# Routing search of an expert network: nine steps for ten, 24 small counting matmuls in the first round, and a new order of VectorE's work in the expert loop

## The chip, the cores and the metric

The kernel runs on one core of one Trainium2 chip. The metric is the device time of one execution in microseconds (us). TensorE (PE) multiplies matrices, with its weight loads shown apart as PEld; VectorE (DVE), ScalarE (ACT) and GpSimd (POOL) do the elementwise work; SyncE (SP) issues most DMAs. Each engine works through its own queue in order, and the queues are tied by semaphores that the program sets and waits for.

## What is computed

Three layers follow one another. A gated linear attention (4 batches, 8 heads, 768 tokens, head size 40) gives x with 3072 rows of 320. A router gives every token one of 8 experts with room for 384 tokens each:

```python
logits = x @ w_gate
order = np.argsort(-logits.flatten())
for idx in order:
    tok, e = (int(idx) // E, int(idx) % E)
    if assigned[tok] >= 0 or counts[e] >= cap:
        continue
    assigned[tok] = e
    counts[e] += 1
for e in range(E):
    mask = assigned == e
    out[mask] = np.maximum(x[mask] @ w1[e], 0.0) @ w2[e]
```

The last layer is the same for all tokens: h = x @ w_in (320 to 2048), g = max(h, 0) + alpha * min(h, 0), y = g @ w_out. All of it is in float32; the large products are made from three matmuls on a high and a low part of each operand.

## The kernel before

**Attention, then a first routing round, then eight experts.** The tokens lie in NT = 24 tiles of 128, T = 4c + b. Attention goes over these tiles. After it the router's greedy order is turned into rounds. A round finds the next expert that becomes full, with its 384 tokens. Round 0 runs alone, before the first expert; round e + 1 runs beside expert e, spread over its hidden tiles. In a round every token has a best open expert; its logit is held as two integers in floats, `route_value` (high bits) and `route_tie` (low bits and the token's place), and `best` finds the maximum of each over the 8 experts and writes the one-hot `choice`.

**One search step.** A threshold is found by ten steps, five on the value and five on the tie (`VALUE_STEPS`, `TIE_STEPS`, each a number of bits and a shift). For a step of 5 bits, `compare` (L1138 without a base, L1140 with one) compares the 24 keys of a partition with 31 thresholds at once, 24 x 31 = 744 results; for 4 bits it is 24 x 15 = 360. `count` (L667) multiplies them with `choice`, four tiles per matmul, six matmuls; `own_blocks` (L1146) keeps the diagonal blocks of the result, `add_four` (L673) adds the partitions, `flag_full` (L1153 to L1155) adds the four columns, compares with the room that is left and gives a flag, and `raise_base` (L679) adds the step to the threshold on all partitions. Then `take` (L1168 on), `close` (L1178 to L1185: who is full, its members, the expert's number in `order`), `rank_members` (L690), `place_members` (L1198 to L1204), three `match_rows` (L1208), `list_tokens` (24 matmuls, L699), `read_tokens` (L1213 to L1217: `idx_in`), `reopen` (L1189 to L1192) and `best` (L1116 to L1120) for the next round.

**What a finished round starts.** SP waits for `order` and loads the expert's weights (L406 to L410). POOL waits for `idx_in` and gathers the expert's rows from DRAM (`fetch_rows`, L532). ACT and DVE split weights and rows into a high and a low part: `high_w1` (L926) with `low_in` (L1246, L1248), `high_w2` (L932) with `low_out` (L1254), and the rows, transposed by PE (`turn_rows`, L720), with `rows_hi` (ACT, L941) and `rows_lo` (DVE, L1258, `xT_lo`). Transposes 1 and 2 use the same PSUM bank as the one before, so each waits until `rows_lo` of that one is done.

**An expert.** Hidden tiles k = 0 to 7 belong to the expert's own layer, k = 8 to 23 to the last layer (j = k - 8). PE makes a hidden tile with `up` (8 matmuls of 384 columns, L726 to L728, L742, L743) and uses it in `down1` or `down2` (9 matmuls). PE runs two hidden tiles ahead: in iteration j it issues `up` of j + 2, then `down2(j)`. For k of 8 or more, ACT makes `g_neg` (L950), DVE `g_act` (L1271), ACT `h_hi` (L952), DVE `h_lo` (L1276), and `down2` waits for that. DVE's work for the routing round and for the next expert's operands is written by hand between these pairs; `split_hidden(e, k)` is the pair, and in the loop over j it is called with k = 8 + j + 2. The text calls the stretch from one `g_act` to the next slot k.

The loop over experts 0 to 6 is one loop in the program; expert 7 has no routing and no successor:

```python
if j + 2 < J2:
    split_hidden(e, J1 + j + 2, ...)
...
if route and j == 10:
    best(ch)
if more and 9 <= j < 12:
    low_in(e + 1, j - 9)
if more and 12 <= j < 15:
    rows_lo(e + 1, j - 12)
if more and 12 <= j < 15:
    low_out(e + 1, j - 12)
```

Of the kernel before, what the change touches and what calls it, by code (L numbers as in the profile page):

```python
# [10 lines left out]
I32 = mybir.dt.int32  # L11
# [23 lines left out]
def build_program(nc, qT, kT, k, v, o, i_gate, f_gate, w_gate, w1, w2, w_in, w_out, alpha, out):  # L35
# [20 lines left out]
    VALUE_STEPS = [(5, 18), (5, 13), (5, 8), (4, 4), (4, 0)]  # L56
    TIE_STEPS = [(5, 19), (4, 15), (4, 11), (4, 7), (4, 3)]
# [10 lines left out]
    with ExitStack() as keep:  # L68
# [217 lines left out]
        above_ready = sem("above_ready")  # L286
        count_ready = sem("count_ready")
# [5 lines left out]
        taken_count = sem("taken_count")  # L293
        keys_ready = sem("keys_ready")
# [265 lines left out]
        def _(pe):  # L560
# [142 lines left out]

            for n in range(NS):
                count(0, n)
                add_four(0, n)
# [43 lines left out]
            def expert(e, more, route):  # L750
# [44 lines left out]
                for j in range(J2):  # L795
                    if j + 2 < J2:
                        up(J1 + j + 2, wi_hi, wi_lo, j + 2, yT_hi, yT_lo,
                           between=(ph, J1 + j - 1) if route and j < 3 else None)
                    if j == J2 - 1 and more:
                        first_up(e + 1)  # L800
                    if route and j < 3:
                        raise_base(ph, J1 + j - 1)
                    if route and j == 4:
# [3 lines left out]
                    if route and j < 2:  # L807
                        count(ph, J1 + j)
                    if route and j == 2:
                        count_taken(ph)  # L810
                    if route and j == 8:
# [21 lines left out]
        def _(act):  # L833
# [120 lines left out]
            def expert(e, more):  # L954
                for k in range(1, JT):
# [25 lines left out]
        def _(dve):  # L981
# [50 lines left out]

            def make_probs(c, b):
# [48 lines left out]
            def step(c, b):  # L1082
# [13 lines left out]
            dve.wait_ge(consts, 8)  # L1096
            ch.link(dve.tensor_copy(add_blocks[:, :], same_step))
            dve.wait_ge(logit_read, NT)
            bits = logits[:, :, :].bitcast(I32)
            ch.link(dve.tensor_scalar(isign[:, :, :], bits, 31, -2 ** 31, ALU.arith_shift_right, ALU.bitwise_or))  # L1100
            ch.link(dve.tensor_tensor(ibits[:, :, :], bits, isign[:, :, :], ALU.bitwise_xor))
            ch.link(dve.tensor_scalar(isign[:, :, :], ibits[:, :, :], 9, None, ALU.logical_shift_right))
            ch.link(dve.tensor_copy(route_value[:, :, :], isign[:, :, :]))
            ch.link(dve.tensor_scalar(ibits[:, :, :], ibits[:, :, :], 511, None, ALU.bitwise_and))
            ch.link(dve.tensor_copy(tmp_a[:, :, :], ibits[:, :, :]))
            ch.link(dve.scalar_tensor_tensor(out=route_tie[:, :, :], in0=tmp_a[:, :, :], scalar=float(2 ** 15), in1=route_tie[:, :, :],
                                             op0=ALU.mult, op1=ALU.add))
            ch.link(dve.memset(need[:, :], float(CAP)))
            ch.link(dve.memset(assigned[:, :, :], 0.0))
# [4 lines left out]
            def best(ch):  # L1114

                ch.link(dve.tensor_reduce(best_value[:, :], route_value[:, :, :], X, ALU.max))  # L1116
                ch.link(dve.tensor_tensor(tmp_a[:, :, :], route_value[:, :, :], bc(best_value[:, :], E), ALU.is_equal))
                ch.link(dve.tensor_tensor(tmp_b[:, :, :], tmp_a[:, :, :], route_tie[:, :, :], ALU.mult))
# [265 lines left out]
```

## Time and profile before

| what | us |
|---|---|
| median of three runs | 900.04 (891.87, 900.04, 902.94) |
| the profiled execution, its own time | 891.99 |
| its span in the trace | 890.1 |
| mean granted clock of TensorE, share of full speed | 0.949 |
| attention, until the last logits are read | 0 to 196.8 |
| first routing round, rows and weights of expert 0 | 196.8 to 248.7 |
| experts 0 to 6, to the first matmul of expert 7 | 248.7 to 810.7 |
| expert 7 and the end | 810.7 to 890.1 |

All times in the rows are microseconds from the start of the span, unless marked ns. A row of the timeline gives start, duration, engine, line, operation, what is written from what, the shapes, and in brackets the engine's idle time before it and what ended it. Two rows that stand close together may overlap: an engine starts the next instruction before the last one has drained.

### The profile page before, as it was taken

The page shows a single profiled execution, that of the slowest core. Times are in us where ns is not written, and L with a number is a line of the kernel's source. Part 1 is how long each engine was busy: PE and PEld are TensorE (multiplying, and loading weights), DVE is VectorE, ACT ScalarE, POOL GpSimd, SP SyncE. Part 2 cuts the span into 40 slices and gives each one's busy share as a digit, 9 for nine tenths or more (in the row PEclk, how much of TensorE's full clock was granted, in tenths as well). Part 3 has the DMA queues.
Part 4 walks back from the last instruction along what each step waited for, and adds up shares of the span by engine and source line. Part 5 has one row for each costly group of instructions (what it writes and reads, how often), then busy time and mean ns, then how long its engine had stood idle before and what let it go on. Part 6 is the DMA issues. An engine that isn't in the chain of part 4 may idle for free.

```text
span 890.1 us, 16834 instructions
## 1 busy us (share of the span) xinstructions
PE 782.2 (88%) x5518; PEld 725.4 (82%) x5518; DVE 597.9 (67%) x1465; ACT 318.0 (36%) x732; POOL 166.9 (19%) x241
## 2 busy tenths in 40 slices
PE   1979999972199989998998999899989989998995
PEld 1878899961088978897897889889978988897995
DVE  7647678856766785777677677767766786775342
ACT  5426555510122441343235134313522441343331
POOL 8427667600100011011001101100110011011001
PEclk9989999975589999999999999999999999999998
DMA  9788887510500400050041005002300400050000
GB/s 250 157 203 193 205 195 173 136 36 1 168 1 1 143 28 23 7 163 22 0 133 35 22 0 159 24 7 67 101 22 0 141 27 22 1 167 23 1 1 22
DMA packets 102510, 68.52 MB, mean 77 GB/s; under 512 B 67984, under 2 KB 92048, under 8 KB 102480
## 3 DMA queue, kind: packets, MB, share of 16 engines
q1 hardware_dynamic: 85872, 45.05, 20.0%
q10 hardware_dynamic: 13920, 14.42, 5.5%
q0 software_dynamic: 2688, 8.65, 3.1%
q8 instruction: 17, 0.28, 0.1%
q14 instruction: 13, 0.11, 0.0%
HBM read 59.46 MB, written 8.65 MB: 77 GB/s over the span
## 4 chain that ended last, share of the span: by engine, by line
PE 51%; DVE 20%; issue 11%; ACT 8%; SPq 4%; DMA 3%; ACTq 1%; POOL 1%; DVEq 0%; POOLq 0%
PE bank L726 12%; PE bank L728 9%; PE bank L727 9%; DVE g_act L1271 6%; ACT h_hi L952 4%; PE bank L595 4%; PE bank L633 4%; PE bank L742 3%; PE bank L743 2%; DMA s<-w 2%; DVE w_lo L1254 2%; PE bank L667 2%; PE bank L617 2%; DVE by_row L1208 1%; PE bank L606 1%
## 5 line engine op out<-in xcount | busy, mean ns | idle before, releaser
L952 ACT CAST h_hi<-g_act 128x384 fp32r<-128x384 f32 x128 | 65.7, 514 | 188.3 <-DVE g_act L1271 188.3
L726 PE MATMUL bank<-wo_hi,h_hi 128*128 128x320 f32 x384 | 122.8, 320 | 0.6 <-DVE h_lo L1276 0.6
L728 PE MATMUL bank<-wo_hi,h_lo 128*128 128x320 f32 x384 | 120.1, 313 | 0.0
L727 PE MATMUL bank<-wo_lo,h_hi 128*128 128x320 f32 x384 | 119.5, 311 | 0.0
L532 POOL DMA_INDIRECT xe<-x_rows,idx_in x24 | 27.9, 1161 | 451.7 <-DVE idx_in L1216 393.3
L1276 DVE TENSOR_TENSOR h_lo<-g_act,h_hi 128x384 fp32r<-128x384 f32 x128 | 71.5, 559 | 59.8 <-ACT h_hi L952 58.0
L1271 DVE SCALAR_TENSOR_TENSOR g_act<-g_neg,rest_alpha,bank 128x384 f32<-128x384 f32 x128 | 78.3, 612 | 21.8 <-ACT g_neg L950 20.6
L726 PE MATMUL bank<-yT_hi,wi_hi 128*128 128x384 f32 x256 | 92.1, 360 | 0.1
L948 ACT ACTIVATE h_hi<-bank 128x384 fp32r<-128x384 f32 x64 | 31.5, 492 | 169.4 <-PE bank L743 169.4
L728 PE MATMUL bank<-yT_hi,wi_lo 128*128 128x384 f32 x256 | 86.6, 338 | 0.0
L727 PE MATMUL bank<-yT_lo,wi_hi 128*128 128x384 f32 x256 | 86.6, 338 | 0.0
L726 PEld LDWEIGHTS bank<-wo_hi,h_hi 128*128 128x128 f32 x384 | 73.4, 191 | 1.0 <-DVE h_lo L1276 0.9
L727 PEld LDWEIGHTS bank<-wo_lo,h_hi 128*128 128x128 f32 x384 | 73.4, 191 | 0.0
L728 PEld LDWEIGHTS bank<-wo_hi,h_lo 128*128 128x128 f32 x384 | 73.3, 191 | 0.0
L950 ACT ACTIVATE g_neg<-bank 128x384 f32<-128x384 f32 x128 | 62.6, 489 | 29.4 <-PE bank L743 28.7
L726 PE MATMUL bank<-h_hi,w_hi 128*128 128x384 f32 x192 | 69.9, 364 | 0.0
L728 PE MATMUL bank<-h_hi,w_lo 128*128 128x384 f32 x192 | 64.7, 337 | 0.0
L727 PE MATMUL bank<-h_lo,w_hi 128*128 128x384 f32 x192 | 64.4, 335 | 0.0
L543 POOL DMA_INDIRECT out<-out_sb,idx_out x24 | 27.3, 1138 | 190.0 <-DVE out_sb L1334 185.1
L861 ACT ACTIVATE decay<-bank,aT 128x128 f32<-128x128 f32 x192 | 51.5, 367 | 13.8 <-PE bank L588 9.6
L595 PE MATMUL bank<-q_wide,k_in 128*128 128x256 f32 x192 | 52.0, 418 | 1.6 <-DVE probs L1039 1.6
L726 PE MATMUL bank<-xT_hi,w_hi 128*128 128x384 f32 x128 | 51.6, 403 | 1.2 <-DVE xT_lo L1258 1.2
(208 smaller groups left out, 1776.8 us busy)
## 6 DMA issues: line engine op xcount, KB each, us to landing
s<-w SPq DMA_DIRECT2D x8, 1280.0 KB, 9.3
s<-w SPq DMA_DIRECT2D x8, 1024.0 KB, 5.4
s<-w SPq DMA_DIRECT2D x24, 256.0 KB, 6.5
sig<-o ACTq DMA_DIRECT2D x6, 640.0 KB, 8.5
q_in<-qT SPq DMA_DIRECT2D x48, 80.0 KB
q_wide<-qT SPq DMA_DIRECT2D x48, 80.0 KB
k_in<-kT SPq DMA_DIRECT2D x48, 80.0 KB
k_row<-k SPq DMA_DIRECT2D x48, 80.0 KB
```

Source lines behind the costliest of these rows:

```text
L532: pool.indirect_dma_start(xe[:, t, :], None, x_rows[:, :], bass.IndirectOffsetOnAxis(ap=idx_in[:, t:t + 1], axis=0)).then_inc(rows_in, 16)
L595: ins = pe.matmul(SCORE[y // 2][:, 2 * P * (y % 2):2 * P * (y % 2) + 2 * P], k_in[:, b, y, :], q_wide[:, b, y, :, :].rearrange("p u t -> p ...
L633: ins = pe.matmul(YB[:, D1 * h:D1 * h + D1], probs[:, n, half, y, :], v_in[:, b, h, :], start=True, stop=True)
L726: pe.matmul(acc, ah, bh, start=start, stop=False, skip_group_check=True)
L727: pe.matmul(acc, ah, bl, start=False, stop=False, skip_group_check=True)
L728: return pe.matmul(acc, al, bh, start=False, stop=stop, skip_group_check=True)
L861: ins = act.activation(decay[:, half, y, :], LOGD[half][:, P * y:P * y + P], ACT.Exp, bias=aT[:, c, h:h + 1])
L948: act.activation(h_hi[:, k % 3, :], acc, ACT.Relu).then_inc(act_ready, 1)
L950: act.activation(g_neg[:, k % 3, :], acc, ACT.Relu, scale=-1.0).then_inc(act_ready, 1)
L952: act.copy(h_hi[:, k % 3, :], g_act[:, k % 3, :]).then_inc(g_hi, 1)
L1271: dve.scalar_tensor_tensor(out=g_act[:, n, :], in0=g_neg[:, n, :], scalar=rest_alpha[:, j:j + 1], in1=acc, op0=ALU.mult, op1=ALU.add).then ...
L1276: dve.tensor_tensor(h_lo[:, n, :], g_act[:, n, :], h_hi[:, n, :].bitcast(F32), ALU.subtract).then_inc(h_ready, 1)
```

## The change

1. The search has nine steps: value (5, 19), (5, 14), (5, 9), (5, 4), (4, 0), tie (5, 18), (5, 13), (5, 8), (5, 3). Eight are of 5 bits, one of 4; before it was four and six.
2. In round 0 alone, a step compares the 24 tiles in two halves of 12 (two instructions), and PE counts with 24 matmuls of 31 weight columns and 8 moving columns into 31 x 8 sums (`first_compare`, `first_count`); the four-tile form and `own_blocks`, `add_four` and the first instruction of `flag_full` are left out there.
3. The conversion of logits to keys and the first `best` are split: 20 of the 24 tiles are done in `early_keys`, put between the last two tiles of attention on DVE; the last four after the last logits.
4. Beside an expert, a round has nine steps, and everything behind the search comes one j earlier on PE and DVE. `best` is cut in two: its value half is done with `reopen` in slot 17 ahead of `read_tokens`, its tie half in slot 18. `turn_rows`, `rows_hi` and `rows_lo` come one j earlier, `low_out` stays at j = 12 and 13, and its third part comes behind `split_hidden` of the next expert's first tile.

```diff
-    VALUE_STEPS = [(5, 18), (5, 13), (5, 8), (4, 4), (4, 0)]
-    TIE_STEPS = [(5, 19), (4, 15), (4, 11), (4, 7), (4, 3)]
+    VALUE_STEPS = [(5, 19), (5, 14), (5, 9), (5, 4), (4, 0)]
+    TIE_STEPS = [(5, 18), (5, 13), (5, 8), (5, 3)]
...
+            def first_count(n):
+                for half in range(2):
+                    pe.wait_ge(halves_ready, 2 * n + half + 1)
+                    for c in range(NT // 2 * half, NT // 2 * half + NT // 2):
+                        ins = pe.matmul(CNT[0:JM, 0:E], above[:, JM * c:JM * c + JM], choice[:, c, :],
+                                        start=(c == 0), stop=(c == NT - 1), skip_group_check=True)
+                ins.then_inc(count_ready, 1)
...
             for n in range(NS):
-                count(0, n)
-                add_four(0, n)
+                first_count(n)
                 raise_base(0, n)
...
-                           between=(ph, J1 + j - 1) if route and j < 3 else None)
+                           between=(ph, J1 + j - 1) if route and j < 2 else None)
...
-                    if more and 12 <= j < 15:
-                        turn_rows(e + 1, j - 12)
+                    if more and 11 <= j < 14:
+                        turn_rows(e + 1, j - 11)
...
+                    if more and 13 <= j:
+                        rows_hi(e + 1, j - 13)
...
-                    if more and 14 <= j:
-                        rows_hi(e + 1, j - 14)
                 if more:
-                    rows_hi(e + 1, 2)
                     activate(e + 1, 0)
...
+                if isinstance(T, int) and T == NT - 2:
+                    early_keys()
...
+            def first_flag(ch, n):
+                J = 2 ** STEPS[n][0] - 1
+                dve.wait_ge(count_ready, n + 1)
+                ch.link(dve.tensor_tensor(hit[0:J, :], CNT[0:J, 0:E], need[0:J, :], ALU.is_ge))
+                dve.tensor_reduce(flag[0:J, :], hit[0:J, :], X, ALU.max).then_inc(flag_ready, 1)
...
-                    if route and j == 9:
+                    if route and j == 8:
                         read_tokens(ch, ph)
...
-                    if route and j == 9:
+                    if route and j == 7:
                         reopen(ch)
-                    if route and j == 10:
-                        best(ch)
+                        choose_value(ch, slice(0, NT))
+                    if route and j == 8:
+                        choose_tie(ch, slice(0, NT))
...
-                    if more and 12 <= j < 15:
-                        rows_lo(e + 1, j - 12)
-                    if more and 12 <= j < 15:
+                    if more and 11 <= j < 14:
+                        rows_lo(e + 1, j - 11)
+                    if more and 12 <= j < 14:
                         low_out(e + 1, j - 12)
                 if more:
                     split_hidden(e + 1, 0)
+                    low_out(e + 1, 2)
```

On DVE, one search step of round 0 before (`by_row` is the memory of the comparisons):

```order
L1140 SCALAR_TENSOR_TENSOR by_row<-best_value,bank,steps 128x744
L1146 TENSOR_TENSOR blocks<-bank,own_block 128x32
L1153 TENSOR_REDUCE cnt_sb<-bank 31x8
L1154 TENSOR_TENSOR hit<-cnt_sb,need 31x8
L1155 TENSOR_REDUCE flag<-hit 31x1
```

And the same step now:

```order
L1195 SCALAR_TENSOR_TENSOR by_row<-best_value,bank,steps 128x372 x2
L1202 TENSOR_TENSOR hit<-bank,need 31x8
L1203 TENSOR_REDUCE flag<-hit 31x1
```

The comparison is in two pieces, and two of DVE's four instructions behind it are gone, with the PE round trip between them. The lines of the changed kernel are numbered anew; L1140 is L1195 there, L1154 is L1202.

On DVE beside an expert, slot 22 and what is ahead of it, before (`w_lo` 1152 is `low_out`, `xT_lo` is `rows_lo`):

```order
L1248 TENSOR_TENSOR w_hi<-s_99,w_hi 64x1024
L1263 REGISTER_ALU
L1271 SCALAR_TENSOR_TENSOR g_act<-g_neg,rest_alpha,bank 128x384
L1275 REGISTER_ALU
L1276 TENSOR_TENSOR h_lo<-g_act,h_hi 128x384
L1257 REGISTER_ALU
L1258 TENSOR_TENSOR xT_lo<-bank,xT_hi 128x384
L1253 REGISTER_ALU
L1254 TENSOR_TENSOR w_lo<-s_100,w_hi 128x1152
L1263 REGISTER_ALU
L1271 SCALAR_TENSOR_TENSOR g_act<-g_neg,rest_alpha,bank 128x384
```

And now:

```order
L1313 TENSOR_TENSOR w_hi<-s_99,w_hi 64x1024
L1322 REGISTER_ALU
L1323 TENSOR_TENSOR xT_lo<-bank,xT_hi 128x384
L1328 REGISTER_ALU
L1336 SCALAR_TENSOR_TENSOR g_act<-g_neg,rest_alpha,bank 128x384
L1340 REGISTER_ALU
L1341 TENSOR_TENSOR h_lo<-g_act,h_hi 128x384
L1322 REGISTER_ALU
L1323 TENSOR_TENSOR xT_lo<-bank,xT_hi 128x384
L1318 REGISTER_ALU
L1319 TENSOR_TENSOR w_lo<-s_100,w_hi 128x1152
```

The first `xT_lo` has moved into slot 21, ahead of `g_act` of slot 22, and the second stands where the first stood.

On PE, the second transpose of the next expert's rows and what is behind it, before (`wo_hi`, `h_hi` are operands of `down2`):

```order
L720 MATMUL bank<-ident,xe 128x128 x3
L726 MATMUL bank<-wo_hi,h_hi 128x320
L727 MATMUL bank<-wo_lo,h_hi 128x320
L728 MATMUL bank<-wo_hi,h_lo 128x320
L726 MATMUL bank<-wo_hi,h_hi 128x320
```

And now:

```order
L731 MATMUL bank<-ident,xe 128x128 x3
L737 MATMUL bank<-yT_hi,wi_hi 128x384
L738 MATMUL bank<-yT_lo,wi_hi 128x384
L739 MATMUL bank<-yT_hi,wi_lo 128x384
L737 MATMUL bank<-yT_hi,wi_hi 128x384
```

Before, `down2(14)` stood behind it; now it is `up` of hidden tile 23, which DVE's slot 23 waits for.

## Rows read from the trace of the kernel before

**Rows 1.** The page's chain of waits: shares of the span by engine.

```profile
PE 51%; DVE 20%; issue 11%; ACT 8%; SPq 4%; DMA 3%; ACTq 1%; POOL 1%; DVEq 0%; POOLq 0%
```

**Rows 2.** PE in the timeline: transposes and last down products of expert 2.

```profile
411.30 0.32 PE L726 MATMUL bank<-wo_hi,h_hi 128*128 128x320 f32 x1
...
485.93 0.55 PE L720 MATMUL bank<-ident,xe 128*128 128x128 f32 x3 [2.48 <-DVE xT_lo L1258]
...
489.32 0.55 PE L720 MATMUL bank<-ident,xe 128*128 128x128 f32 x3 [1.53 <-DVE xT_lo L1258]
...
491.51 0.31 PE L726 MATMUL bank<-wo_hi,h_hi 128*128 128x320 f32 x1
```

**Rows 3.** DVE in the timeline, slots 10 to 23 of that expert.

```profile
446.76 0.62 DVE L1271 SCALAR_TENSOR_TENSOR g_act<-g_neg,rest_alpha,bank 128x384 f32<-128x384 f32 x1
...
449.97 0.61 DVE L1271 SCALAR_TENSOR_TENSOR g_act<-g_neg,rest_alpha,bank 128x384 f32<-128x384 f32 x1
...
455.63 0.61 DVE L1271 SCALAR_TENSOR_TENSOR g_act<-g_neg,rest_alpha,bank 128x384 f32<-128x384 f32 x1
...
457.30 0.61 DVE L1271 SCALAR_TENSOR_TENSOR g_act<-g_neg,rest_alpha,bank 128x384 f32<-128x384 f32 x1
...
470.87 0.17 DVE L1216 CAST idx_in<-token_f 128x3 int32<-128x3 f32 x1
...
471.48 0.62 DVE L1271 SCALAR_TENSOR_TENSOR g_act<-g_neg,rest_alpha,bank 128x384 f32<-128x384 f32 x1 [0.31 <-ACT g_neg L950]
...
485.31 0.56 DVE L1258 TENSOR_TENSOR xT_lo<-bank,xT_hi 128x384 fp32r<-128x384 f32 x1 [0.55 <-ACT xT_hi L941]
...
488.71 0.55 DVE L1258 TENSOR_TENSOR xT_lo<-bank,xT_hi 128x384 fp32r<-128x384 f32 x1
489.18 1.35 DVE L1254 TENSOR_TENSOR w_lo<-s,w_hi 128x1152 fp32r<-128x1152 f32 x1
490.44 0.55 DVE L1258 TENSOR_TENSOR xT_lo<-bank,xT_hi 128x384 fp32r<-128x384 f32 x1
...
492.23 0.56 DVE L1266 SCALAR_TENSOR_TENSOR h_lo<-bank,h_hi 128x384 fp32r<-128x384 f32 x1 [0.37 <-ACT h_hi L948]
```

**Rows 4.** DVE in the timeline: end of attention, last logits, first comparison of round 0.

```profile
186.91 0.49 DVE L1079 TENSOR_TENSOR x_sb<-scaled,sig 128x320 f32<-128x320 f32 x1
190.79 0.50 DVE L1059 TENSOR_TENSOR carried<-bank,gT 128x328 f32<-128x328 f32 x1 [3.38 <-PE bank L633]
...
196.73 0.17 DVE L1097 CAST add_blocks<-tmp_a 128x31 fp32r<-128x31 f32 x1
...
201.50 0.94 DVE L1138 TENSOR_TENSOR by_row<-best_value,steps 128x744 bf16<-128x744 f32 x1
```

**Rows 5.** Timeline of both engines, second step of round 0, and the step's neighbours.

```profile
204.23 1.00 DVE L1140 SCALAR_TENSOR_TENSOR by_row<-best_value,bank,steps 128x744 bf16<-128x744 f32 x1 [0.28 <-PE bank L679]
205.28 0.34 PE L667 MATMUL bank<-choice,by_row 128*128 128x32 bf16 x6 [1.09 <-DVE by_row L1140]
...
207.02 1.00 DVE L1140 SCALAR_TENSOR_TENSOR by_row<-best_value,bank,steps 128x744 bf16<-128x744 f32 x1 [0.28 <-PE bank L679]
...
209.81 0.60 DVE L1140 SCALAR_TENSOR_TENSOR by_row<-best_value,bank,steps 128x360 bf16<-128x360 f32 x1 [0.28 <-PE bank L679]
...
227.52 0.42 DVE L1168 SCALAR_TENSOR_TENSOR taken<-key,bank,choice 128x192 bf16<-128x192 f32 x1 [0.28 <-PE bank L679]
```

**Rows 6.** PE in the timeline: eight small bf16 matmuls, and six f32 ones of the router.

```profile
235.47 0.37 PE L699 MATMUL bank<-by_tile,by_row 128*128 128x6 bf16 x8 [0.76 <-DVE by_row L1208]
...
192.14 1.42 PE L606 MATMUL bank<-wg_sb,xT_sb 128*128 128x8 f32 x6 [0.71 <-ACT xT_sb L869]
```

**Rows 7.** Stretches of the span: us, busy of PE, PEld, DVE, ACT, POOL, PEclk, DMA share, GB/s.

```profile
406.00:408.00 2.00, 2.00 (x10) 1.92 (x8) 1.42 (x3) 0.75 (x2) 0.00 (x0) 0.51 0.00 0
477.00:478.00 1.00, 1.00 (x8) 1.00 (x7) 0.90 (x4) 0.74 (x2) 0.00 (x0) 1.00 0.33 123
478.00:479.00 1.00, 1.00 (x8) 1.00 (x7) 0.84 (x3) 0.00 (x0) 0.00 (x0) 1.00 0.00 0
```

More of the change, by code:

```diff
@@ L1095, in _ @@
             ch = Chain(dve, dve_step, gate_steps + STEP_LINKS * NT - B)
[L1096 to L1109, printed above, removed]
+            dve.wait_ge(key_step, KEY_LINKS)
+            make_keys(ch, slice(NT - B, NT))
+            choose(ch, slice(NT - B, NT))
+            links0 = ch.base + ch.n
             def e_first(ap):
@@ L1114, in best @@
             def best(ch):
[L1116 to L1123 removed]
+                choose(ch, slice(0, NT))
             LINKS = 27 + 2 * NS
@@ L1141, in compare, with first_compare @@
                                              in1=st, op0=ALU.subtract, op1=ALU.is_ge).then_inc(above_ready, 1)
+            def first_compare(n):
+                J = 2 ** STEPS[n][0] - 1
+                tie = n >= len(VALUE_STEPS)
+                key = key2 if tie else best_value
+                base = TIE_BASE if tie else VALUE_BASE
+                if n not in (0, len(VALUE_STEPS)):
+                    dve.wait_ge(base_ready, n)
+                for half in range(2):
+                    cs = slice(NT // 2 * half, NT // 2 * half + NT // 2)
+                    st = steps[:, n, 0:J].unsqueeze(1).to_broadcast([P, NT // 2, J])
+                    if n in (0, len(VALUE_STEPS)):
+                        dve.tensor_tensor(above_chunks(J)[:, cs, :], bc(key[:, cs], J), st, ALU.is_ge).then_inc(halves_ready, 1)
+                    else:
+                        dve.scalar_tensor_tensor(out=above_chunks(J)[:, cs, :], in0=bc(key[:, cs], J), scalar=base,
+                                                 in1=st, op0=ALU.subtract, op1=ALU.is_ge).then_inc(halves_ready, 1)
+            def first_flag(ch, n):
+                J = 2 ** STEPS[n][0] - 1
+                dve.wait_ge(count_ready, n + 1)
+                ch.link(dve.tensor_tensor(hit[0:J, :], CNT[0:J, 0:E], need[0:J, :], ALU.is_ge))
+                dve.tensor_reduce(flag[0:J, :], hit[0:J, :], X, ALU.max).then_inc(flag_ready, 1)
             def own_blocks(ch, ph, n):
@@ L1228, in _ @@
                     keys_at_value(ch, 0)
-                compare(ch, 0, n)
-                own_blocks(ch, 0, n)
-                flag_full(ch, 0, n)
+                first_compare(n)
+                first_flag(ch, n)
+            dve.sem_inc(blocks_ready, NS)
+            dve.sem_inc(above_ready, NS)
+            dve.sem_inc(dve_step, NS)
+            ch.n += NS
             take(ch, 0)
@@ L1303, in expert @@
                 for j in range(J2):
-                    if route and j < 2:
+                    if route and j < 1:
                         own_blocks(ch, ph, J1 + j)
                         flag_full(ch, ph, J1 + j)
-                    if route and j == 3:
+                    if route and j == 2:
                         close(ch, ph)
-                    if route and j == 9:
+                    if route and j == 8:
                         read_tokens(ch, ph)
                     if j + 2 < J2:
-                        split_hidden(e, J1 + j + 2, ((compare, ch, ph, J1 + 1) if j == 0 else (take, ch, ph)) if route and j < 2 else None)
-                    if route and j == 4:
+                        split_hidden(e, J1 + j + 2, (take, ch, ph) if route and j == 0 else None)
+                    if route and j == 3:
                         place_members(ch, ph)
-                    if route and 5 <= j < 8:
-                        match_rows(ch, ph, j - 5)
-                    if route and j == 9:
+                    if route and 4 <= j < 7:
+                        match_rows(ch, ph, j - 4)
+                    if route and j == 7:
                         reopen(ch)
-                    if route and j == 10:
-                        best(ch)
+                        choose_value(ch, slice(0, NT))
+                    if route and j == 8:
+                        choose_tie(ch, slice(0, NT))
                     if more and 9 <= j < 12:
                         low_in(e + 1, j - 9)
-                    if more and 12 <= j < 15:
-                        rows_lo(e + 1, j - 12)
-                    if more and 12 <= j < 15:
+                    if more and 11 <= j < 14:
+                        rows_lo(e + 1, j - 11)
+                    if more and 12 <= j < 14:
                         low_out(e + 1, j - 12)
```

46 lines of the change are left out of this document (38 added, 8 removed).

## The prediction

> **What bounds the kernel now.** I read the chain of waits first: half of it is PE, and some 28% is DVE and ACT [rows 1]. The timeline tells where. Round 0 of the routing, 196.7 to 227.5, is one serial chain, DVE for the most part, with nothing beside it [rows 4, 5]. Beside an expert PE works without a gap until it meets the transposes of the next expert's rows. There it waits 2.48 and then 1.53 us, both times for DVE's `xT_lo` [rows 2]. One expert, from last down product to last down product, takes 491.51 - 411.30 = 80.21 us [rows 2], seven times over. DVE comes late to these transposes since its slots are full: a slot with nothing extra takes 457.30 - 455.63 = 1.67 us, and the fourteen from 446.76 to 492.23 take 45.47 us, 3.25 each [rows 3], where PE needs about 2.7 for an up and a down product. So round 0 is bound by its chain, and the tail of every expert by what stands in DVE's queue ahead of `xT_lo`.
>
> **Round 0: the keys.** Before, conversion and first `best` took 201.50 - 196.73 = 4.77 us for 17 instructions [rows 4]. Behind the last logits 12 stay, 32 results wide. Nearest is the 31-wide copy, 0.17 us, 0.21 with its step to the next [rows 4]: 12 x 0.21 = 2.5. That gives 2.25 us. The 15 early instructions are 160 wide instead of 192; scaled from the 4.77 they take about 4.4. They start when DVE issues the last `x_sb`, about 187.4, and DVE was idle only 3.38 us until 190.79 [rows 4]. So they end near 191.8, and the last tile of attention, on which the last logits hang, starts 0.9 late (bounds 0.5 and 1.5). Net gain 1.35 us.
>
> **Round 0: the search.** A step of 5 bits takes 207.02 - 204.23 = 2.79 us; all ten take 227.52 - 201.50 = 26.02, with 0.65 of it for the tie's keys [rows 5]. Now, per step of 5 bits:
> 744 results take 1.00 and 360 take 0.60 [rows 5], so a result costs 1.04 ns and a half of 372 takes 0.61. Two independent halves overlap by about 0.08: 1.14 us. The 12 matmuls of the first half lie beside the second compare. Those of the second half are open: eight small bf16 matmuls take 0.37 us at the low clock [rows 6], 0.04 for each further one, so 0.53 for twelve, 0.05 to start and 0.03 to DVE. The two instructions that stay and `raise_base` take, from the same step, 0.20 + 0.21 + 0.22. Sum 2.38 us, 0.41 less than before. The 4-bit step comes to 1.99, the two first steps of each kind (no base, 0.94 for 1.00) to 2.27. Nine steps: 2 x 2.27 + 6 x 2.38 + 1.99 = 20.8, with the keys 21.5. Gain 4.5 us. The weights' load, the gather and all behind them hang on this chain, so it moves everything forward: 5.85 us with the keys.
>
> Bounds of the small matmul: 0.04 us (the bf16 row) and 0.24 us (the router's six f32 ones took 1.42 [rows 6]). I take 0.04, since operands and size are those of that row. The Trainium skill (TensorE: Matmul & The Clock Gate, "Back-to-back issue gap") speaks against it: it gives about 81 ns for each pair of weight load and matmul at N = 128. By that the second half would take about 0.45 us more in each of nine steps, and the forecast would be 4 us higher; an estimate. The trace's row is of the smaller N that is used here, so it decides.
>
> **Beside an expert: what DVE loses and keeps.** Slots 0 to 9 keep their pace: there a step is paced by PE, and it costs PE about 0.5 us (count, add, raise and the breaks between them). The compares that grow from 360 to 744 results cost DVE 0.40 each, in slots where DVE waited for PE's counts; if that cover were gone it would be 3 x 0.4 per expert. From slot 10 to the first `h_lo` of the next expert these go from DVE's chain:
> - the tenth step: slot 10 took 449.97 - 446.76 = 3.21, 1.54 more than a bare one [rows 3]. Close, place, match and list move up one slot, with unchanged prices.
> - the wait for ACT's `g_neg` in slot 18, 0.31 [rows 3]: `best`'s halves and `read_tokens` now fill slots 17 and 18, and ACT is ready before DVE.
> - the wait of the first `xT_lo` for ACT, 0.55 [rows 3]: it now stands a slot earlier, with `low_in` ahead of it, and PE transposed long before.
> - the third `low_out`: from 490.44 to 492.23 less `xT_lo` (489.18 - 488.71 = 0.47) and the idle 0.37 is 0.95; the idle 0.37 goes as well [rows 3]. It is now ahead of the three copies of `out_sb`, which free the banks for the next expert's first `down1`. They end some 3.2 us behind the start of the last down product, about when PE has finished that and one up product (2.7 us) and asks for the first of them. Covered, with half a us to spare at most.
>
> Sum 1.54 + 0.31 + 0.55 + 0.95 + 0.37 = 3.72 us. Seen from PE: the first `xT_lo` starts at 485.31 less 1.85 (the two first), less 0.55, less 1.67 (one slot earlier) = 481.24 and ends at 481.8. PE then has transposes, an up and down product (2.7), and what it did from 485.93 to 491.51 without idle (5.58 - 1.53 - 0.4), 6.35 together, so the last down product starts at 488.15, 3.4 us earlier. Between 3.4 and 3.9 I take 3.7: 7 x 3.7 = 26 us. PE would still wait about 1.4 us at the second transpose.
>
> **Sum.** 891.99 is the profiled execution's own time. 891.99 - 5.85 - 26 = 860.1. The three runs of before lie at 891.87, 900.04 and 902.94: the profile is of the fast end, the median 8 us above. I expect the same scatter after and put the forecast at 862.
>
> **What the moved steps start.** `idx_in` is written at 470.87 and the gather's traffic is over by 478.0, since the stretch 477 to 478 has a share of 0.33 and the next none [rows 3, 7]: 7.1 us. Now it is written about 469.0, so the rows are there at 476.1. The first transpose stands near 477.1. Slack 1.0 us on PE, about 2 before DVE feels it. The weights' load starts a slot earlier too and ends earlier.
>
> **Rivals.**
> A. The rows or transposes come late. The second transpose now stands ahead of `up` of tile 23, so a PE that waits there also holds up DVE's slot 23; before, only down products were behind it. If the gather needs 2 us more than now, or ACT's share of the rows is late, each us is lost once per expert, and what stays is PE's 0.5 for the step: 892 - 5.85 - 3.5 = 882.7. Against it stand the slacks just counted, 1 to 2 us.
> B. PE is the bound after all. All of its idle (2.48 + 1.53, and about 0.9 of slow starts) goes, and the step's 0.5: 5.4 x 7 = 38, so 848. Against it: DVE's chain from slot 10 is still 41.7 us long.
> C. The clock. In 406 to 408 the granted clock was 0.51, at 1.2 GHz after the idle of 2.5 us [rows 7], and it cost nothing, as PE waited anyhow. Where PE no longer waits, such a stretch costs half its length; I bound it by 1.7 us, for one that reaches a little past both ends of this row. In every expert: 860 + 12 = 872. Against it: the waits shrink to half.
> D. Slower. The 24 small matmuls with a new weight load each run at the router's 0.24 us. Then no half hides, and a step takes 0.66 + 24 x 0.24 + 0.63 = 7.05, nine of them with the keys 63.9 for 26.0: 892 - 1.35 + 37.9 - 26 = 902.5, 1.2% slower. It decides from (26.0 + 27.3) / 9 = 5.9 us per step on, that is 0.19 us per matmul. Against it: bf16 at 0.04 in the same phase at the same low clock [rows 6].
>
> **How the numbers follow.** The forecast 0.72, A 0.10, B 0.08, C 0.06, D 0.04. Faster by over 2% (below 882 against 900; 2% is about what a measurement of this kernel tells from no change) are the forecast, B, C: 0.86. A lies at the edge and D within 2%; with a D that comes out dearer the chances are 0.12 for same and 0.02 for slower. The range: below, B's floor, 848 less the chance that the round's gain is larger, 847; above, C with the 8 us of scatter, 880. The forecast alone has 852 to 872.
>
> **What would show it.** Right: ten compares of round 0 replaced by nine pairs at a pitch of 2.4 us, the expert's period 76.5, one wait of about 1.4 us at the second transpose and nearly none at the third, `carried` of the last tile 0.9 late. Wrong: a period above 78, PE idle at the first transpose behind the gather, or small matmuls above 0.1 us each.

## The result, and the profile after

| | before | after |
|---|---|---|
| median, us | 895.95 (891.48 to 902.94, 4 runs) | 864.48 (863.09 to 866.06, 4 runs) |
| ratio | | 0.9642, 95% interval 0.9564 to 0.9721 |
| profiled execution, us (span) | 891.99 (890.1) | 865.21 (861.9) |
| `x_sb` of tile 22, us | 186.91 | 190.18 |
| from there to the first matmul of expert 0 | 61.74 | 57.28 |
| experts 0 to 6, us each | 80.29 | 76.49 |
| from the first matmul of expert 7 to the end | 79.4 | 79.0 |

The kernel is 3.6% faster. The forecast was 862, with a range of 847 to 880. Profile against profile, 26.8 us went: 26.6 in the seven tails, 4.5 in round 0 and 0.4 at the end, less 3.3 that attention took longer, and less 1.4 by which the time outside the span grew (1.9 before, 3.3 after).

PE in the timeline of the kernel after, the three transposes and the first of the last down products of expert 1. They answer to [rows 2]; L731 is L720 of before.

```profile
391.24 0.49 PE L731 MATMUL bank<-ident,xe 128*128 128x128 f32 x3
...
395.81 0.55 PE L731 MATMUL bank<-ident,xe 128*128 128x128 f32 x3 [1.38 <-DVE xT_lo L1323]
...
398.91 0.49 PE L731 MATMUL bank<-ident,xe 128*128 128x128 f32 x3
...
401.94 0.31 PE L737 MATMUL bank<-wo_hi,h_hi 128*128 128x320 f32 x1
```

The two waits of 2.48 and 1.53 us have become one of 1.38, at the second transpose. The first waits for nothing, so the gathered rows are there; nor does the third. The same product of the expert before stands at 325.46, so an expert takes 401.94 - 325.46 = 76.48 us. All seven lie between 76.43 and 76.59. A third stop of PE in before, beside those of [rows 2], is gone too. It is shorter, and lies ahead of the last two matmuls of the next expert's first `up`, which need the third `xT_lo`:

```profile
490.58 0.34 PE L728 MATMUL bank<-xT_hi,w_lo 128*128 128x384 f32 x1
491.05 0.45 PE L742 MATMUL bank<-xT_hi,w_hi 128*128 128x384 f32 x1
```

From the start of that `up` to the last down product it was 491.51 - 489.62 = 1.89 us; it is 401.94 - 400.55 = 1.39 now.

DVE in the same stretch, answering to [rows 3]:

```profile
383.40 0.17 DVE L1278 CAST idx_in<-token_f 128x3 int32<-128x3 f32 x1
...
395.20 0.56 DVE L1323 TENSOR_TENSOR xT_lo<-bank,xT_hi 128x384 fp32r<-128x384 f32 x1
395.67 0.60 DVE L1336 SCALAR_TENSOR_TENSOR g_act<-g_neg,rest_alpha,bank 128x384 f32<-128x384 f32 x1
...
397.33 0.55 DVE L1323 TENSOR_TENSOR xT_lo<-bank,xT_hi 128x384 fp32r<-128x384 f32 x1
```

The first `xT_lo` has lost its idle time ahead (0.55 before), and the second follows 2.13 us behind it where it took 3.40 (488.71 - 485.31).

One step of round 0, timeline of both engines, answering to [rows 5]:

```profile
206.60 1.13 DVE L1195 SCALAR_TENSOR_TENSOR by_row<-best_value,bank,steps 128x372 bf16<-128x372 f32 x2 [0.28 <-PE bank L690]
207.26 1.01 PE L678 MATMUL bank<-choice,by_row 128*31 128x8 bf16 x24 [0.70 <-DVE by_row L1195]
208.31 0.15 DVE L1202 TENSOR_TENSOR hit<-bank,need 31x8 f32<-31x8 f32 x1 [0.58 <-PE bank L678]
208.50 0.15 DVE L1203 TENSOR_REDUCE flag<-hit 31x1 bf16<-31x8 f32 x1
208.71 0.19 PE L690 MATMUL bank<-flag,step_size 128*128 128x1 bf16 x1 [0.43 <-DVE flag L1203]
208.93 0.61 DVE L1195 SCALAR_TENSOR_TENSOR by_row<-best_value,bank,steps 128x372 bf16<-128x372 f32 x1 [0.28 <-PE bank L690]
```

A step takes 208.93 - 206.60 = 2.33 us for 2.79. Behind the second half of the comparison DVE sits idle 0.58 us, which is the start and run of twelve small matmuls, at the low clock: some 0.04 us each.

### The profile page after: what moved, and what is told of

It reads as the page before. It is cut to its first block, busy times and chain, and to the rows that moved or that the text cites. A ratio compares the mean times of both kernels' runs of the same rounds, so it can differ in the third digit from the quotient of the medians.

```text
span 861.9 us, 16958 instructions
## 1 busy us (share of the span) xinstructions
PE 776.5 (90%) x5607; PEld 726.4 (84%) x5607; DVE 596.4 (69%) x1427; ACT 316.9 (37%) x732; POOL 167.5 (19%) x240
## 4 chain that ended last, share of the span: by engine, by line
PE 54%; DVE 20%; issue 9%; ACT 6%; SPq 4%; DMA 2%; POOL 1%; ACTq 1%; DVEq 0%; POOLq 0%
PE bank L737 12%; PE bank L739 10%; PE bank L738 10%; DVE g_act L1336 6%; ACT h_hi L963 5%; PE bank L597 4%; PE bank L635 4%; PE bank L753 2%; PE bank L754 2%; PE bank L619 2%; DVE w_lo L1311 2%; PE bank L608 1%; DMA s<-w 1%; PE bank L669 1%; DVE by_row L1270 1%
## 5 line engine op out<-in xcount | busy, mean ns | idle before, releaser
L737 PE MATMUL bank<-wo_hi,h_hi 128*128 128x320 f32 x384 | 120.8, 315 | 0.6 <-DVE h_lo L1341 0.6
L534 POOL DMA_INDIRECT xe<-x_rows,idx_in x24 | 23.3, 972 | 426.8 <-DVE idx_in L1278 373.8
L545 POOL DMA_INDIRECT out<-out_sb,idx_out x24 | 30.7, 1277 | 183.1 <-DVE out_sb L1401 178.2
```

What stands on the lines that cost most here:

```text
L545: pool.indirect_dma_start(out[:, :], bass.IndirectOffsetOnAxis(ap=idx_out[:, t:t + 1], axis=0), out_sb[:, t, :], None).then_inc(out_sent, 16)
L737: pe.matmul(acc, ah, bh, start=start, stop=False, skip_group_check=True)
```

## The experiments

Ten kernels were run in all, the two of the change and eight variants. The table has their medians and, from their traces, the usual time of an expert with the wait at each transpose. Each ratio is to runs of the kernel of before made beside that variant's own, and their median moved: 895.95 us for after, 901.73 for e1 to e4, 894.45 for e5 to e8. So medians of different rows are compared to about 5 us only; what an edit is worth is read from the experts' times.

| kernel | median us | ratio to before, interval | us per expert | waits at transposes 1, 2, 3 |
|---|---|---|---|---|
| before | 895.95 | | 80.2 to 80.5 | 0, 2.48, 1.53 (0.3 to 0.6 in every second expert, where the clock has fallen) |
| after | 864.48 | 0.9642 (0.9564 to 0.9721) | 76.5 | 0, 1.38, 0 |
| e1_old_tail | 873.04 | 0.9717 (0.9657 to 0.9776) | 78.17 | 0, 0.91, 1.53 |
| e2_tail_only | 882.44 | 0.9814 (0.9753 to 0.9876) | 78.5 | 0.54, 2.18, 0 |
| e3_rows_first | 861.38 | 0.9583 (0.9521 to 0.9645) | 76.33 | 0, 0, 0.24, and 0.49 behind them |
| e4_low_out_inside | 861.57 | 0.9580 (0.9521 to 0.9639) | 76.45 | 0, 1.35, 0 |
| e5_keys_late | 864.27 | 0.9626 (0.9569 to 0.9684) | 76.46 | 0, 1.35, 0 |
| e6_old_count | 866.55 | 0.9660 (0.9602 to 0.9718) | 76.58 | 0, 1.48, 0 |
| e7_tokens_late | 877.11 | 0.9758 (0.9694 to 0.9821) | 77.4 to 80.5 | 2.3 to 2.7, 0, 0 |
| e8_low_out_out_of_tail | 859.51 | 0.9574 (0.9517 to 0.9631) | 76.0 | 0, 0, 0.25 |

### The tail's order taken back, and put in alone

e1_old_tail, on the kernel after:

```diff
-                    if more and 11 <= j < 14:
-                        turn_rows(e + 1, j - 11)
+                    if more and 12 <= j < 15:
+                        turn_rows(e + 1, j - 12)
...
-                    if more and 11 <= j < 14:
-                        rows_lo(e + 1, j - 11)
-                    if more and 12 <= j < 14:
+                    if more and 12 <= j < 15:
+                        rows_lo(e + 1, j - 12)
+                    if more and 12 <= j < 15:
                         low_out(e + 1, j - 12)
                 if more:
                     split_hidden(e + 1, 0)
-                    low_out(e + 1, 2)
```

with `rows_hi` on ACT one j later as well.

> The changed kernel with the tail of each expert in the order of before: transposes, rows_hi and rows_lo one j later, the third low_out ahead of the next expert's first split_hidden. Nine steps, the earlier routing and round 0 stay. Theory of the prediction (DVE's chain is a sum of its pieces): the step's 1.54 us and ACT's 0.31 stay saved, 1.87 us come back, so an expert takes 76.5 + 1.9 = 78.4 us and the whole 864.5 + 13 = 877.5 us. Rival (the earlier routing alone frees the tail, the order behind it is idle play): an expert stays below 77 us and the whole below 868 us.

Measured: 78.17 us per expert, where 78.4 was expected, and 8.6 us more in the medians, where 13 was. The experts make 7 x 1.68 = 11.8 of it; in the profiled execution `x_sb` of tile 22 came 3.1 us earlier than in after (187.04 for 190.18). PE in the timeline of this run, transposes 2 and 3 of expert 1:

```profile
394.67 0.55 PE L731 MATMUL bank<-ident,xe 128*128 128x128 f32 x3 [0.91 <-DVE xT_lo L1324]
...
398.06 0.55 PE L731 MATMUL bank<-ident,xe 128*128 128x128 f32 x3 [1.53 <-DVE xT_lo L1324]
```

The third transpose waits 1.53 us again, as in [rows 2]; the second waits 0.91 for 2.48. So the step that is gone and the earlier routing are worth 80.29 - 78.17 = 2.1 us per expert (1.85 by the prediction's terms), and the tail's order 78.17 - 76.49 = 1.7 (1.87). The rival falls.

e2_tail_only is the same edit the other way round, on the kernel before.

> The kernel of before, ten steps and all, with the tail's new order alone: transposes, rows_hi and rows_lo one j earlier, the third low_out behind split_hidden. Theory of the prediction: 1.87 us per expert go, 80.3 - 1.9 = 78.4 us each, 13 us in all, about 883 us against 896. Rival (with the routing late the gathered rows miss the earlier transpose, and PE waits there for the DMA): an expert takes 79.7 us or more, the whole 892 or more.

Measured: five experts of 78.5 us and two of 80.61 and 80.01; the median is 882.44, where 883 was expected. That match says little, as the runs of before made beside it have a median of 901.73; the experts' times are the evidence. The order alone gives 1.8 us per expert, so the two parts (2.1 and 1.7 or 1.8) add up to the 3.8 of the change. The rows do come late for the earlier transpose, by 0.54 us, and it costs little. The two long experts are those in which TensorE's clock fell. Stretches of this run, with the columns of [rows 7]; the first two are in the long experts, the third in one of 78.5:

```profile
323.00:326.40 3.40, 3.40 (x14) 3.36 (x13) 2.82 (x5) 1.80 (x4) 0.00 (x0) 0.51 0.00 0
401.60:404.90 3.30, 3.10 (x11) 3.10 (x12) 2.72 (x5) 1.65 (x3) 0.00 (x0) 0.50 0.00 0
481.00:485.00 4.00, 3.19 (x21) 3.19 (x22) 3.39 (x6) 2.16 (x5) 0.00 (x0) 1.00 0.00 0
```

The fall followed PE's waits of 2.17 and 2.29 us at the second transpose; in the other five experts the wait there was 2.17 to 2.22 us and the clock stayed. Here PE has an `up` behind that wait: at half clock it does 14 matmuls in 3.40 busy us and 11 in 3.10, at full clock 21 in 3.19. The experts are 2.1 and 1.5 us longer (the first is expert 0, which also begins at the low clock). So 1.5 us is the price of rival C, which the prediction bounded by 1.7.

### The third low_out back inside

```diff
                     if more and 11 <= j < 14:
                         rows_lo(e + 1, j - 11)
-                    if more and 12 <= j < 14:
+                    if more and 12 <= j < 15:
                         low_out(e + 1, j - 12)
                 if more:
                     split_hidden(e + 1, 0)
-                    low_out(e + 1, 2)
```

> The changed kernel with the third low_out (0.95 us on DVE) back ahead of the next expert's first split_hidden. By the prediction's sum, which credits its move with 0.95 and the idle with 0.37 on the path, an expert takes 0.95 to 1.3 us more, the whole 7 to 9 us more (872). Rival: PE's last down product waits only for the third xT_lo and h_lo of tile 23, both ahead of this instruction, and the next down1 asks for h_lo 2.7 us later; then nothing changes: 76.5 us per expert, within 1 us of 864.5.

Measured: 76.45 us per expert, the same waits, 861.57. PE in the timeline, the second transpose of expert 1 in this run:

```profile
397.09 0.55 PE L731 MATMUL bank<-ident,xe 128*128 128x128 f32 x3 [1.35 <-DVE xT_lo L1323]
```

The move of the third `low_out` is worth nothing. The median is even 2.9 us lower than that of after; no expert accounts for that, and the stretch ahead of them scatters by as much (below).

### The first xT_lo earlier still, and the tail made shorter

e3_rows_first:

```diff
-                    if more and 9 <= j < 12:
-                        low_in(e + 1, j - 9)
                     if more and 11 <= j < 14:
                         rows_lo(e + 1, j - 11)
+                    if more and 9 <= j < 12:
+                        low_in(e + 1, j - 9)
```

> The changed kernel with the first xT_lo ahead of the third low_in in slot 21 of DVE (1.35 us earlier); nothing else. PE's wait of 1.38 us at the second transpose shrinks to less than 0.2 in both theories. If that wait is what is left of the bound, an expert takes 75.2 to 75.4 us and the whole 856 us. If DVE's chain up to the third xT_lo and the next expert's first up product is what bounds (it is no shorter, and ends only about 0.3 us before PE asks for it), PE waits there instead, and an expert takes 76.1 to 76.3 us, the whole 862 us.

Measured: the wait of 1.38 us is gone, and an expert takes 76.33 us, 0.15 less. PE in the timeline, the three transposes of expert 1 in this run:

```profile
389.32 0.49 PE L731 MATMUL bank<-ident,xe 128*128 128x128 f32 x3
...
392.53 0.55 PE L731 MATMUL bank<-ident,xe 128*128 128x128 f32 x3
...
396.04 0.55 PE L731 MATMUL bank<-ident,xe 128*128 128x128 f32 x3 [0.24 <-DVE xT_lo L1323]
...
399.43 0.45 PE L753 MATMUL bank<-xT_hi,w_hi 128*128 128x384 f32 x1 [0.49 <-DVE xT_lo L1323]
```

A wait of 1.38 us was worth 0.15. PE now waits for the second `xT_lo` at the third transpose (from the second to the third 3.51 us for 3.10), and the last line is a new wait, for the third `xT_lo`, in the next expert's first `up`. In after that matmul starts at 401.59, 0.3 us behind the end of the third `xT_lo` (400.73 + 0.55), and waits for nothing. DVE's chain to the third `xT_lo` is as long as before, and PE had that 0.3 us to spare. The theory of the chain holds.

e8_low_out_out_of_tail takes `low_out` out of that chain (for expert 0, too, the third one moves into its own layer):

```diff
                     if more and 11 <= j < 14:
                         rows_lo(e + 1, j - 11)
+                    if more and 9 <= j < 12:
+                        low_in(e + 1, j - 9)
-                    if more and 12 <= j < 14:
-                        low_out(e + 1, j - 12)
+                    if more and j == 13:
+                        low_out(e + 1, 0)
                 if more:
                     split_hidden(e + 1, 0)
-                    low_out(e + 1, 2)
+                    low_out(e + 1, 1)
...
                     split_hidden(e, k)
+                    if k == 5:
+                        low_out(e, 2)
```

> The changed kernel with DVE's tail made shorter ahead of the third xT_lo: first xT_lo ahead of the third low_in; first low_out in slot 23 behind the third xT_lo, second behind the next expert's first split_hidden, third in the next expert's own layer behind hidden tile 5. If DVE's chain up to the third xT_lo is what bounds (theory of the run with the rows first), PE becomes the bound: no waits at the transposes and 75.1 to 75.5 us per expert, the whole 855 to 857 us. Rival: the moved pieces make DVE late for the copies of out_sb or for a count of the search, and the 1.2 us come back there: 76.3 us, the whole 862.

Measured: 76.0 us per expert and 859.51, between the two. Its median is the lowest, 0.9574 of before, though the intervals of e3 and e4 overlap with it; against after it is 5 us lower, of which 7 x 0.49 = 3.4 lie in the experts. Two delays are left, PE first, then DVE's copy of `out_sb`, both at expert 1:

```profile
398.41 0.55 PE L731 MATMUL bank<-ident,xe 128*128 128x128 f32 x3 [0.24 <-DVE xT_lo L1323]
...
404.56 0.45 PE L737 MATMUL bank<-h_hi,w_hi 128*128 128x384 f32 x1
404.85 0.34 PE L738 MATMUL bank<-h_lo,w_hi 128*128 128x384 f32 x1
```

```profile
402.76 1.35 DVE L1319 TENSOR_TENSOR w_lo<-s,w_hi 128x1152 fp32r<-128x1152 f32 x1
404.02 1.28 DVE L1403 COPY out_sb<-bank 128x320 f32<-128x320 f32 x3
```

The third transpose still waits 0.24 us for the second `xT_lo`, so from the second transpose to the third PE takes 3.51 us for 3.10 in after. And the first `down1` of the next expert starts late: from the last down product to its second matmul 404.85 - 401.56 = 3.29 us, for 404.85 - 401.94 = 2.91 in after. It needs the bank that the first of the three copies of `out_sb` frees (one copy takes 0.48 us, so from 404.02 to 404.50), and the second `low_out`, 1.35 us, now stands ahead of that copy where a piece of 0.95 stood. That is the place of the rival. The two delays are 0.4 us each; without them the expert would be at 75.2, inside the theory's 75.1 to 75.5 (an estimate from these rows).

### The tokens one slot later

```diff
-                    if route and j == 8:
+                    if route and j == 9:
                         read_tokens(ch, ph)
```

> The changed kernel with read_tokens one slot later (j = 9), so the gather of the next expert's rows starts 2.8 us later. Theory of the slacks (1.0 us on PE, about 2 before DVE feels it): PE waits about 2 us for the DMA at the first transpose, its wait at the second shrinks, and an expert takes 0.4 to 0.8 us more: 868 us. Rival A of the prediction (each us of lateness is lost once per expert, as the transposes now stand ahead of an up product): 2 us or more per expert, 878 us and above.

Measured: 877.11. PE in the timeline, first and second transpose of expert 1 in this run:

```profile
398.71 0.55 PE L731 MATMUL bank<-ident,xe 128*128 128x128 f32 x3 [2.32 <-DMA xe<-x_rows,idx_in]
401.82 0.49 PE L731 MATMUL bank<-ident,xe 128*128 128x128 f32 x3
```

PE waits 2.32 us for the gather and nothing at the second transpose. `idx_in` is written at 391.44 here, so the rows take 398.71 - 391.44 = 7.27 us. In after the first transpose stands 391.24 - 383.40 = 7.84 us behind `idx_in`: the slack on PE is 0.6 us, where the prediction counted 1.0. This expert takes 77.4 us, 0.9 more than in after: the wait mostly took the other's place, a little more dearly than the 0.4 to 0.8 expected. But in four of the seven experts the clock fell during or behind the new wait, and they take 79.0 to 80.5 (the longest is expert 0, which also begins at the low clock). Two stretches of this run, in the tails of experts 2 and 4, with the columns of [rows 7]:

```profile
478.00:480.00 2.00, 2.00 (x8) 2.00 (x7) 0.56 (x1) 1.03 (x1) 0.00 (x0) 0.53 0.00 0
634.00:636.00 2.00, 2.00 (x8) 2.00 (x7) 1.18 (x2) 1.12 (x2) 0.00 (x0) 0.50 0.00 0
```

The total came near what rival A had named (878 and above), by C's mechanism: a wait of 2.3 us for the rows costs 1 us by itself and 1.5 to 2 us more where the clock falls with it.

### Round 0

e5_keys_late: without `early_keys`, all 24 tiles' keys behind the last logits.

```diff
-                if isinstance(T, int) and T == NT - 2:
-                    early_keys()
...
-            dve.wait_ge(key_step, KEY_LINKS)
-            make_keys(ch, slice(NT - B, NT))
-            choose(ch, slice(NT - B, NT))
...
+            make_keys(ch, slice(0, NT))
+            choose(ch, slice(0, NT))
```

> The changed kernel without early_keys: all 24 tiles' keys and the first best behind the last logits, as before. Read from the stretch between x_sb of tile 22 and the first comparison. If the early keys hold up the last tile on DVE: from the last logits to the comparison 4.8 us for 2.8, and the last tile 0.6 us shorter, net +1.4 us of 864.5. Rival: they hide wholly beside PE, net +2.0 us. A stretch in which TensorE's granted clock falls earlier or later moves the last tile by 1 to 2 us by itself and is to be told apart by PE's idle before carried.

Measured: from the last logits to the first comparison 205.51 - 201.09 = 4.42 us (4.8 expected), for 204.40 - 201.61 = 2.79 in after: 1.63. The median, 864.27, doesn't tell them apart. Whether the early keys hold up the last tile depends on the clock. DVE in the timeline, `x_sb` of tile 22 and `carried` of tile 23, first in e5_keys_late, then in e1_old_tail, which has the early keys:

```profile
190.67 0.49 DVE L1131 TENSOR_TENSOR x_sb<-scaled,sig 128x320 f32<-128x320 f32 x1
195.23 0.50 DVE L1111 TENSOR_TENSOR carried<-bank,gT 128x328 f32<-128x328 f32 x1 [4.07 <-PE bank L635]
```

```profile
187.04 0.49 DVE L1132 TENSOR_TENSOR x_sb<-scaled,sig 128x320 f32<-128x320 f32 x1
...
191.13 0.33 DVE L1066 TENSOR_TENSOR choice<-tmp_b,best_tie 128x160 bf16<-128x160 f32 x1
191.49 0.50 DVE L1112 TENSOR_TENSOR carried<-bank,gT 128x328 f32<-128x328 f32 x1
```

In e1_old_tail `carried` follows the last early key at once, 4.45 us behind `x_sb`, for 3.88 in [rows 4]: 0.57 late. e6_old_count shows the same 4.45. In e5_keys_late there are no early keys, and the distance is 4.56, of which DVE idles 4.07 waiting for PE. The granted clock had fallen by the time of that `x_sb` (0.64 from 190 to 192, 0.50 from then on), where in before it fell 0.7 us behind it (0.90 from 186 to 188), so PE did more of the last tile slowly. There the early keys would hide whole, as in after, where DVE waited 1.17 us for PE.

e6_old_count: nine steps, round 0 counted as before.

```diff
-            pe.sem_inc(four_ready, NS)
             for n in range(NS):
-                first_count(n)
+                count(0, n)
+                add_four(0, n)
                 raise_base(0, n)
...
-                first_compare(n)
-                first_flag(ch, n)
+                compare(ch, 0, n)
+                own_blocks(ch, 0, n)
+                flag_full(ch, 0, n)
```

> The changed kernel with nine steps, but round 0 counted as before: one comparison of all tiles, six matmuls of four tiles, own_blocks, add_four, three instructions of flag_full. The prediction's prices: a step of 5 bits takes 2.79 us again for 2.33, the search 25.2 us for 21.0, the whole 4.2 us more, 868.7. Then the step that is gone is worth nothing by itself in round 0 (26.0 against 25.2, since four steps grow from 4 to 5 bits). Rival (small matmuls cost as much as they save, the gain is the ninth step's): the search stays within 1 us of 21.

Measured: the search takes 227.00 - 201.78 = 25.22 us, for 20.99 in after and 26.02 before. DVE in the timeline of this run:

```profile
204.50 1.00 DVE L1178 SCALAR_TENSOR_TENSOR by_row<-best_value,bank,steps 128x744 bf16<-128x744 f32 x1 [0.28 <-PE bank L690]
...
207.29 1.00 DVE L1178 SCALAR_TENSOR_TENSOR by_row<-best_value,bank,steps 128x744 bf16<-128x744 f32 x1 [0.28 <-PE bank L690]
```

A step takes 2.79 us again. Of the 5.0 us that round 0's search gained, 4.2 are the new way of counting and 0.8 the step that is gone. In the medians 2.1 us of the 4.2 show. The profiled execution has the rest: against after, its last tile of attention, from `x_sb` of tile 22 to that of tile 23, was 1.1 us shorter (6.69 for 7.81), and from `idx_in` to the first matmul of expert 0 it took 0.9 us less (12.61 for 13.51).

### The kernel of before, four executions more

Its runs lie in two groups, near 893 us at a mean granted clock of 0.945 and near 901 us at 0.932, with one at 897.5 between them. Four more executions were profiled; the kernel is unchanged.

> The kernel of before, unchanged, looked at once more. Its runs lie in two groups, near 893 us with a mean granted clock of 0.945 and near 901 us with 0.932. Theory: in the second group TensorE's clock falls in more tails, or at a place in the tail where PE is busy behind its waits; such an expert takes 1.5 us more (81.5 to 82 us for 80.2), and some five of seven together make the 8 us. Rival: the 8 us lie in attention or in the routing round, and the experts take 80.2 to 80.5 us each in both groups.

> As the first further look at the kernel of before: experts of 80.2 us where the clock does not fall or falls wholly within PE's waits, of 81.5 to 82 us where it falls behind them (theory), or 80.2 to 80.5 us throughout with the difference ahead of the first expert (rival).

> A third further look at the kernel of before, in search of an execution near 901 us (the two looked at took 891). Theory: such a one has experts of 81.5 to 82 us, where TensorE's clock falls behind the waits; rival: the 8 us lie ahead of the first expert.

> A fourth further look at the kernel of before, with the same question: where the 8 us between its two groups of runs lie, in experts of 81.5 to 82 us (theory) or ahead of the first expert (rival).

They took 891.16, 891.69, 893.77 and 893.15 us. None fell in the slower group, so the question is not settled. In all four the experts from 2 on take 80.1 to 80.3 us, with the clock falling in or beside PE's waits in every second tail. In the last two expert 0 takes 81.3 and 81.5. In b3_before_again it begins at the low clock for longer: 1.0 us more than in before to its first transpose (71.84 for 70.84). In b4_before_again the clock fell in its tail, and behind the waits:

```profile
326.00:328.00 2.00, 1.56 (x7) 1.57 (x8) 2.00 (x3) 0.18 (x1) 0.00 (x0) 0.50 0.00 0
330.00:332.00 2.00, 2.00 (x8) 2.00 (x9) 1.76 (x3) 0.48 (x1) 0.00 (x0) 0.50 0.00 0
```

From its first transpose to its last down product that tail takes 332.73 - 320.18 = 12.55 us, for 330.86 - 319.49 = 11.37 in before: 1.2 us. So what the theory says of one expert occurs and has about its price; that it makes up the 8 us is not shown.

## Why the prediction was right, point by point

**The place.** PE's waits for `xT_lo` at the transposes were the bound; they shrank as said (one wait of "about 1.4 us", measured 1.38), and the expert took 76.49 us, 3.8 less, for the 3.7 of the forecast. Of the 3.8, 3.1 are PE's waits: 2.48, 1.53 and 0.5 before, 1.38 after.

**The sum of DVE's terms was wrong in its makeup.** It credited 0.95 us to the third `low_out` and 0.37 to the idle behind it. e4_low_out_inside shows the first at nothing, since what PE's last down product waits for, the third `xT_lo` and slot 23, stands ahead of it; the idle stands behind the same two and can count for no more. What carried the 1.7 us of the order is where the transposes, `rows_hi` and `xT_lo` stand, the only difference left between e1_old_tail (78.17) and e4_low_out_inside (76.45). Without the two terms the sum has 0.55 us for the order, so that 3.72 came close to 3.8 is luck. The second way of reckoning, from PE, had no such term and gave 3.4; its way, from DVE's `xT_lo` to what PE does behind it, is the one that the runs bear out. The step's part, 1.85, measured 2.1.

**Round 0's search.** 21.5 us forecast, 20.99 measured; 2.38 a step, 2.33 measured. The small matmuls run at the price of the bf16 row of [rows 6]. Rival D falls, and so does the estimate that was worked out from the 81 ns of the Trainium skill, which are given for N = 128: twelve weight loads and matmuls of this smaller size fit in 0.58 us.

**The keys.** Net 1.35 us forecast. The stretch behind the last logits fell by 2.06 (2.25 forecast), and `carried` is late by 0.57 (0.9 forecast) or not at all, depending on the clock. In the profiled execution part of it was lost again: from `x_sb` of tile 22 to that of tile 23 took 1.69 us longer (7.81 for 6.12), with DVE waiting for PE at the low clock and not for the keys, and the last weights landed 0.95 us later after their issue (11.01 for 10.06). So 5.03 of the search and 2.06 of the keys, less 1.69 and 0.94, leave 4.46 us of the 5.85.

**The rivals.** A: the rows were in time, by 0.6 us, and e7_tokens_late shows about 1 us lost for a wait of 2.3 us, until the clock joins in. B: the floor of 5.4 us below 80.2 that the prediction drew for PE was not reached; with 1.35 us less ahead of the first `xT_lo` and `low_out` out of the way the expert only fell to 76.0. The prediction left the copies of `out_sb` "half a us to spare at most"; in after it is 0.2 (first copy done at 404.48, asked for at 404.67), and e8_low_out_out_of_tail used it up. C did not occur in after, whose clock stays full through all seven experts once it is back near the start of the first; e2_tail_only gives its price.

**What was missed.** Attention took longer, and the scatter did not stay. The forecast took 860.1 for the profiled execution (865.21 measured): attention took 3.3 us more, round 0 gave 1.4 less, the time outside the span grew by 1.4, and experts and end gave 1.0 more. It added 2 for a scatter of 8 us like before's. After's four runs lie within 3 us. These errors partly cancel in 862 against 864.48, so that closeness is luck in part.

## What to carry to other kernels

Price the removal of an instruction from the queue of the engine that is waited for only if it stands ahead of what the waiter asks for; one behind it was worth nothing here (0.95 us on DVE moved in e4_low_out_inside, no change), however full the engine is. It can still delay the next thing that is asked for, as the copies of `out_sb` in e8_low_out_out_of_tail. A wait that can be seen is an upper bound: 1.38 us of it gone gave 0.15, as the next one was close behind. And a wait of 2.2 to 2.7 us on TensorE cost 1.5 us or more beyond itself in the tails in which the granted clock fell to 0.5 and an `up` stood behind it.

## What the runs showed that was not expected

Attention is longer in every kernel made from the changed one, though its code there is the same but for the early keys. `x_sb` of tile 22 starts between 185.5 and 186.9 in six profiles with the old step tables (before, its four repetitions, e2_tail_only) and between 187.0 and 192.2 in eight with the new ones, e5_keys_late without early keys and e6_old_count with the old count among them. The means are 186.3 and 190.0. It begins at tile 4. PE in the timeline there, before and after:

```profile
53.69 1.03 PE L588 MATMUL bank<-peak,sel 128*128 x8 [4.91 <-DMA v_in<-v]
```

```profile
56.01 1.03 PE L590 MATMUL bank<-peak,sel 128*128 x8 [6.54 <-DMA v_in<-v]
```

PE waits 6.54 us for tile 4's loads, where it waited 4.91; this matmul starts between 52.3 and 53.7 in the first set and between 55.1 and 56.5 in the second. Of the 2.3 us between the two lines, 1.2 lie in the issue of the load (46.08 for 44.85) and 1.1 in its landing (9.69 for 8.60). Tile 6's `x_sb` then starts at 80.1 against 83.2 in the means of the two sets. What the kernels of the second set share is the number of steps, which also makes one table in SBUF smaller, and the routing one slot earlier beside the experts. Whether the place of the tensors in SBUF, the length of the programs or something else delays the loads was not tried. It took back 3.3 us of the gain in the profiled execution.
